# Attention scores of the tail in two parts, other slots for loads and splits, and scores directly behind the transposes in TensorE's order

## The reference

```
attention, batch 4, 8 heads, 576 positions, head width 64:
  cum    = cumsum(max(s, 0))
  scores = q k^T / 8 + min(cum_j - cum_i, 0), masked above the diagonal
  x      = softmax(scores) v                       -> 2304 tokens x 512
first MLP, 512 -> 1024 -> 512:
  h    = x w_in;  solu = h * softmax(h)
  x2   = ((solu - mean) / sqrt(var + 1e-6) * g_ln) w_out
second MLP, 512 -> 2048 -> 512:
  h2   = x2 w2_in;  out = (h2 * clip(h2 + 3, 0, 6) / 6) w2_out
```

## Time and profile before

| | |
|---|---|
| runs | 983.62 and 980.97 us, median 982.3 |
| profiled execution | 981.87 us, its span 980.1 us |
| TensorE busy | 868.6 us (89%), weight loads 772.0 us (79%) |
| VectorE, ScalarE, GpSimd busy | 432.1, 409.5, 309.0 us |
| granted TensorE clock, mean | 0.956 of full speed |
| moved by DMA | 66.60 MB, mean 68 GB/s |

### The profile page before, as it was taken

One profiled execution on the slowest core, in us unless ns is written; L12 is line 12 of the kernel. 1 busy time (PEld: TensorE's weight loads), 2 busy tenths in 40 slices (PEclk: granted clock), 3 DMA queues, 4 the chain that ended last, 5 costly groups with the idle time before them and its releaser, 6 DMA issues.

```text
span 980.1 us, 13896 instructions
## 1 busy us (share of the span) xinstructions
PE 868.6 (89%) x4912; PEld 772.0 (79%) x4912; DVE 432.1 (44%) x1059; ACT 409.5 (42%) x901; POOL 309.0 (32%) x419
## 2 busy tenths in 40 slices
PE   5865778988788998888898899999999999999997
PEld 4654567777777887777887799999999999999996
DVE  3545656656566554666564423223223222222222
ACT  5545655455565454655532324332222222222222
POOL 5884365444563444644426414300000000000000
PEclk9988859999999998999999999999999999999999
DMA  6638223343333333433212204000000000000000
GB/s 186 174 103 220 83 83 93 93 104 99 102 101 92 86 87 105 116 88 97 56 57 74 87 1 129 1 33 1 1 33 1 33 1 1 33 1 1 33 1 32
DMA packets 42724, 66.60 MB, mean 68 GB/s; under 512 B 8032, under 2 KB 20320, under 8 KB 42656
## 3 DMA queue, kind: packets, MB, share of 16 engines
q1 hardware_dynamic: 42656, 65.71, 24.3%
HBM read 60.90 MB, written 4.79 MB: 67 GB/s over the span
## 4 chain that ended last, share of the span: by engine, by line
PE 74%; DVE 8%; issue 6%; ACT 6%; POOL 4%; DMA 1%; SPq 1%; ACTq 0%; DVEq 0%; POOLq 0%
PE psum L737 10%; PE psum L766 7%; PE psum L788 7%; PE psum L786 7%; PE psum L787 7%; PE psum L804 7%; PE psum L805 7%; PE psum L803 7%; PE psum L707 5%; PE psum L682 3%; PE psum L663 3%; PE psum L668 2%; DVE es L944 2%; ACT es L1099 2%; PE psum L750 1%
## 5 line engine op out<-in xcount | busy, mean ns | idle before, releaser
L1011 DVE SCALAR_TENSOR_TENSOR act<-act,psum 128x384 f32<-128x384 f32 x96 | 53.2, 554 | 288.8 <-ACT act L1155 288.8
L1155 ACT ACTIVATE act<-psum,three 128x384 f32<-128x384 f32 x96 | 55.7, 580 | 289.1 <-PE psum L788 289.1
L663 PE MATMUL psum<-qk_hi 128*128 128x128 f32 (+2 forms) x192 | 70.0, 370 | 70.0 <-issue 29.4
L1057 ACT ACTIVATE prob<-prob,nmax 128x128 f32<-128x128 f32 (+4 forms) x144 | 83.6, 581 | 113.1 <-DVE nmax L875 112.9
L786 PE MATMUL psum<-x_hi,w_hi 128*128 128x384 f32 x384 | 130.0, 339 | 0.0
L788 PE MATMUL psum<-x_hi,w_lo 128*128 128x384 f32 x384 | 130.0, 339 | 0.0
L787 PE MATMUL psum<-x_lo,w_hi 128*128 128x384 f32 x384 | 129.5, 337 | 0.0
L805 PE MATMUL psum<-w_hi,g_lo 128*128 128x512 f32 x288 | 113.9, 395 | 0.0
L804 PE MATMUL psum<-w_lo,g_hi 128*128 128x512 f32 x288 | 113.7, 395 | 0.0
L803 PE MATMUL psum<-w_hi,g_hi 128*128 128x512 f32 x288 | 112.0, 389 | 0.0
L547 POOL TENSOR_TENSOR qk_hi<-qk_raw,qk_hi 64x256 fp32r<-64x256 f32 (+1 forms) x64 | 55.9, 873 | 169.2 <-ACT qk_hi L1049 167.7
(11 more groups left out here) (92 smaller groups left out, 1931.4 us busy)
## 6 DMA issues: line engine op xcount, KB each, us to landing
qk_raw<-qk SPq DMA_DIRECT2D x64, 240.0 KB, 4.3
qk_raw<-qk SPq DMA_DIRECT2D x64, 128.0 KB, 2.8
bias<-cum_dram SPq DMA_DIRECT2D x32, 256.0 KB, 3.5
bias_tail<-cum_dram SPq DMA_DIRECT2D x32, 144.0 KB, 4.1
out<-out_sb SPq DMA_DIRECT2D x6, 768.0 KB, 3.5
bias<-cum_dram SPq DMA_DIRECT2D x32, 128.0 KB, 3.2
v_raw<-v_main SPq DMA_DIRECT2D x32, 128.0 KB, 2.2
w_raw<-w_in SPq DMA_DIRECT2D x16, 256.0 KB, 3.2
```

What stands on the lines that cost most here:

```text
L663: pe.matmul(ps, q, qk_hi[p][:, keys], start=(e_ == heads[0]), stop=False)
L1057: sc.activation(p, p, ACT.Exp, scale=-1.0, bias=nmax[:, u % 2, col:col + 1], accum_out=rsum[:, u % 2, col:col + 1]).then_inc(exp_done, 1)
```

## The change

- **Tail in two parts.** `scores` gets a `part`. Part 0 (head 0 of the tail, with the mask, opening the accumulation) is made directly behind the scores of item 2, part 1 (head 1, closing it) in the tail's own place. A new semaphore `tail_half_ready` tells that head 0's tile is free, and its next load waits for that alone.
- **Banks.** Item 2 of a second-kind unit goes to bank 0 in place of 2. Only scores in bank 2 still wait for the last tail's p_lo.
- **Splits.** Head 0 of a unit is split at `BASE - 3`, and at `BASE - 4` for the places 5 to 7; head 1 at `BASE - 2` everywhere (before: `BASE - 1` for the second kind and for place 0).
- **Loads.** Each head's array holds q and k twice in DRAM, so that one DMA fills 128 partitions in place of two of 64; v is padded to 640 rows, so that its second load and VectorE's two memsets go. SyncE issues the loads of q and k ahead of the biases.
- **Orders.** TensorE: transposes, scores, scales, values, then all of the slot's filler in one piece. VectorE: row maximum first, maximum and SOLU of the MLP behind the attention's steps. ScalarE: the MLP's exponential in step 4 and Square in step 5, both ahead of the slot's other work (before: steps 3 and 4, behind it). GpSimd: `widen` a slot later, variance behind the splits of v. The split of x comes up to one slot earlier.

```diff
-S_BANKS = [((2 * (u % PAIRS) + k) % 3,) if FIRST_KIND[u] else ((0,), (1,), (2,), (0,), (1, 2))[k] for u, k in ITEM]
+S_BANKS = [((2 * (u % PAIRS) + k) % 3,) if FIRST_KIND[u] else ((0,), (1,), (0,), (0,), (1, 2))[k] for u, k in ITEM]
...
-    SPLIT_AT.setdefault(BASE[_u] - 3, []).append((_u, 0))
-    SPLIT_AT.setdefault(BASE[_u] - (2 if FIRST_KIND[_u] and _u % (2 * PAIRS) else 1 if _u else 2), []).append((_u, 1))
+    SPLIT_AT.setdefault(BASE[_u] - (3 if _u % (2 * PAIRS) <= PAIRS else 4), []).append((_u, 0))
+    SPLIT_AT.setdefault(BASE[_u] - 2, []).append((_u, 1))
...
-X_AT = {STARTS[t] - 2: t for t in range(NT)}
+X_AT = {max(STARTS[t] - 3, whole_at(t)): t for t in range(NT)}
+SPLIT_X_AT = {n + 1: t for n, t in X_AT.items()}
...
@@ SyncE @@
-                    sp.wait_ge(scores_ready, BASE[u_] + (e_ if FIRST_KIND[u_] else 4) + 1)
+                    if FIRST_KIND[u_] or e_ == 1:
+                        sp.wait_ge(scores_ready, BASE[u_] + (e_ if FIRST_KIND[u_] else 4) + 1)
+                    else:
+                        sp.wait_ge(tail_half_ready, sum(not k for k in FIRST_KIND[:u_ + 1]))
-                for half in (slice(0, DH), slice(DH, P)):
-                    sp.dma_start(qk_raw[p][half, 0:w], src).then_inc(qk_loaded[p], 16)
+                sp.dma_start(qk_raw[p][:, 0:w], (qk1, qk0)[c][head_of(u, e)]).then_inc(qk_loaded[p], 16)
...
@@ TensorE, scores @@
-                if S_BEFORE[n] >= 0:
+                if part != 1 and S_BEFORE[n] >= 0:
                     pe.wait_ge(max_done, TILES_BEFORE[S_BEFORE[n] + 1])
-                    if ITEM[S_BEFORE[n]][1] == 4:
-                        pe.wait_ge(pT_lo_done, LOS_BEFORE[S_BEFORE[n] + 1])
-                    elif 2 in S_BANKS[n] and any(ITEM[m][1] == 4 for m in range(max(0, n - 5), n)):
...
+                if part != 1 and 2 in S_BANKS[n]:
+                    m = max([m for m in range(n) if ITEM[m][1] == 4], default=-1)
+                    wait(pe, pT_lo_done, LOS_BEFORE[m + 1])
...
+                last.then_inc(tail_half_ready if part == 0 else scores_ready, 1)
...
@@ TensorE, the slot @@
             for n in range(-2, END):
+                if 0 <= n < ITEMS:
+                    transpose_probs(n)
+                if 0 <= n + 2 < ITEMS:
+                    k = ITEM[n + 2][1]
+                    if k == 4:
+                        scores(n + 2, 1)
+                    else:
+                        scores(n + 2)
+                    if k == 2:
+                        scores(n + 4, 0)
                 if n in SCALES_AT:
                     scales(SCALES_AT[n])
                 for u, e in SUMS_AT.get(n, ()):
                     weighted_values(u, e)
-                if 0 <= n < ITEMS:
-                    transpose_probs(n)
...
-                if 0 <= n + 2 < ITEMS:
-                    scores(n + 2)
...
```

More of the change, by code:

```diff
@@ L476, in _ @@
             for n in range(-2, BASE[UNITS] + 4):
+                for load in range(3, 2 * UNITS):
+                    u_, e_ = (load - 3) // 2, (load - 3) % 2
+                    if BASE[u_] + (e_ if FIRST_KIND[u_] else 2 * e_ + 2) == n + 2:
+                        load_qk(load // 2, load % 2)
                 for u in range(2, UNITS):
@@ L487, in _ @@
                             load_bias_tail(u)
[L488 to L491, removed]
                 for u in range(2, UNITS):
@@ L620, in _ @@
                     behind = split_v(u, e)
+                if r == 5:
+                    behind = variance(t)
                 for u, e in SPLIT_AT.get(n, ()):
@@ L655, in scores @@
                     diag0 = tile * P
-                    heads = (0, 1) if e is None else (e,)
+                    p = load_of(u, part if e is None else e) % 3
+                    q = qk_hi[p][:, q_at:q_at + P]
                     for lo_, hi_ in [(0, w)] if w <= BANK else [(0, w // 2), (w // 2, w)]:
                         ps = psum[:, at + lo_:at + hi_]
[L659 to L669, removed]
+                        keys = slice(QW[c] + lo_, QW[c] + hi_)
+                        pe.matmul(ps, q, qk_hi[p][:, keys], start=(part != 1), stop=False)
+                        if hi_ > diag0 and part != 1:
+                            mask = mask_tail if e is None else mask_bf
+                            pe.matmul(psum[:, at + diag0:at + hi_], ident_bf[:, :], mask[:, 0:hi_ - diag0],
+                                      start=False, stop=False)
+                        last = pe.matmul(ps, q, qk_lo[p][:, keys], start=False, stop=(part != 0))
+                last.then_inc(tail_half_ready if part == 0 else scores_ready, 1)
             def transpose_probs(n):
@@ L974, in _ @@
                 t, r = STEP_AT.get(n, (None, None))
+                if 0 <= n + 1 < ITEMS:
+                    for tile, e, col in TILES[n + 1]:
+                        row_max(n + 1, tile, e, col)
                 if r == 0 and t >= 3:
                     copy_x2(2 * (t - 3) + 1)
+                if 0 <= n < ITEMS:
+                    split_probs(n)
+                if r == 4 and t >= 2:
+                    copy_x2(2 * (t - 2))
+                if n in SCALES_AT:
+                    scale_pair(SCALES_AT[n])
+                for u, e in SUMS_AT.get(n, ()):
+                    add_parts(u, e)
+                for u in range(UNITS):
+                    if BASE[u + 1] == n:
+                        invert(u)
                 if r == 3:
@@ L1128, in _ @@
                 t, r = STEP_AT.get(n, (None, None))
-                sums = n in SUMS_AT
-                if 0 <= n < ITEMS and not sums:
+                if r == 4:
+                    exp1(t)
+                if r == 5:
+                    square(t)
+                if 0 <= n < ITEMS:
                     copy_probs(n)
```

68 lines of the change are left out of this document (22 added, 46 removed).

## The result

The changed kernel takes 1014.8 us (1014.52 to 1015.12, two runs) against 982.3 us; the ratio is 1.0331, with a 95% interval of 1.027 to 1.0392. The forecast was 944 us with a range of 908 to 984: wrong in sign.

The account below looks back on a forecast made before the run. TensorE's waits, mostly before the scores' first matmuls, were taken to bound the kernel, with GpSimd setting the first 64 us. Terms summed to -38 us, from a median of 982.3 to 944 us; range 908 to 984.

Parts of the forecast that it names:

- G: TensorE's attention slots: scales, values and transposes, behind the scores or waiting for earlier scores' exponentials, wait less: -5 us.
- D: Scores directly behind the transposes lose the cover of other matmuls, so first-kind scores wait for splits: +10 us, bounds 0 and +25.
- E: Items k=2 and k=3 share bank 0, so scores of k=3 wait for k=2's row maximum: +8 us, bounds 0 and +23.
- I: ScalarE's MLP exponential and Square ahead of probabilities' copies, VectorE's maximum and SOLU last, delay attention: +12 us, bounds 0 and +40.
- V: Follow-up theory, not a forecast step: values products behind the scores hold p_hi, making ScalarE's copy and everything behind it late.
- A: Head 0 split one slot earlier for units behind another second-kind unit; most 384-column score waits go: -16.6 us.
- B: Scores no longer wait for the tail's p_lo in bank 1 (512-column form): -10.6 us, bounds -5 and -10.6.
- C: Tail's half 0 in slot k=0 lets head 1 load and split earlier; three waits at batch ends go: -12.2 us.
- F: Projection waits for VectorE's copy shrink: -6 us between 64 and 498 us, -6 us in the stretch without attention.
- H: TensorE's clock between 64 and 498 us: a third of 28 us lost comes back, -10 us, bounds 0 and -22.
- The start: First stretch: two loads less for SyncE and splits a slot earlier, -2 us, bounds 0 and -8.
- the third: Rival, slower: scores' waits for splits or maxima are paid in full, filler queued behind; 1013 us, chance 0.07.

Follow-up runs that it names:

- e14: e9 with ScalarE's copy of the probabilities held, in 15 of the same slots, until TensorE has made the slot's scores: 1004.0 us.
- e9: Changed kernel with only the 16 values products of second-kind units' head 0 moved between transposes and scores: 978.0 us.
- e6: Changed kernel with TensorE's scales and values products moved between transposes and scores, all filler still behind the scores: 946.9 us.
- e13: Changed kernel with item k=2 back in bank 2, the tail's half 0 behind the scores of k=3, and head 1's load a slot later: 997.5 us.
- e8: e2 with item k=2 back in bank 2, the tail's half 0 behind the scores of k=3, and head 1's load a slot later: 925.8 us.
- e2: Changed kernel with TensorE's slot as transposes, scales, values, half the filler, scores, other half of the filler: 927.6 us.
- e10: e2 with the heads' splits in the slots of the kernel before; loads, tail and banks as in e2: 952.6 us.
- e11: e2 with the wait for the tail's p_lo put back before the scores that follow a tail in bank 1: 937.7 us.
- e7: e2 with VectorE's and ScalarE's slots in the order of the kernel before: 955.0 us.
- e5: Changed kernel with TensorE's, VectorE's and ScalarE's orders of the kernel before: 953.8 us (952.9 us with only TensorE's order of before).

## Why the prediction was wrong, step by step

**The step that failed is G.** It counted "scales, values and transposes come behind the scores" as a gain of 5 us. I looked at what TensorE waits for there (the scales' own 4.4 us), and not at what the moved products release: p_hi for ScalarE's copy in the same slot (26 us by e14, with 11 us more in e9), and ScalarE's copy of the products, behind which the conversions of the heads are queued (31 us by e9 against e6 for all remaining products and scales; that this path carries them is read from the trace). The line was in the kernel, `sc.wait_ge(pv_done, 2 * (u - 1) + k // 2 + 1)`, and its wait had cost next to nothing only since the products were the first work of the slot. Moving the products from behind the scores to ahead of them, with nothing else touched, takes 1014.8 to 946.9 us, which is the forecast of 944 within 3 us. That is in part luck: there D costs more than its term, E less, and I is no loss, as below. The shared bank of E takes 17 of these 68 us, but only since the maxima are late (e13 against e8).

**E** had the right place and wait, at 8 us; the scores of k = 3 wait 18.1 us on nmax in the changed kernel, within the bound of 23, and the tail's halves another 5.8, which the step had not foreseen. The size came from V: with the products ahead all nmax waits are 3.2 us (e6), and 0.4 in e2.

**D** was forecast at +10 over the waits of before, for lost cover at the first kind's scores; e6 against e2 measures 19 us for the cover of all scores. By form the first kind waits 31.8 us where the step had 20, again with the late products in it. The first kind's waits in e2 are 6.1 us:

```profile
L668 PE MATMUL psum<-qk_hi 128*128 128x512 f32 x29 | 12.3, 424 | 0.4 <-DVE nmax L884 0.4
...
L668 PE MATMUL psum<-qk_hi 128*128 128x384 f32 x28 | 9.9, 352 | 1.9 <-issue 1.9
...
L668 PE MATMUL psum<-qk_hi 128*128 128x128 f32 x24 | 6.4, 268 | 6.1 <-POOL qk_hi L555 4.5 <-issue 1.6
```

**A, B, C** held, once the products are out of the way. In e2 the 384-column form waits 1.9 us, the 512-column form 0.4, and no wait at a batch's end is over 1.4 us. Steps A and C together (-28.8) measure 25 us (e10), B (-10.6) 10 us (e11); by the ratios, which take out the chip, 28 and 13 us. In the changed kernel the 384-column form is still at 9.4 us; a head's conversion stands behind ScalarE's late copies there, but no run tells this apart.

**F** put 0.65 us on a place: in the changed kernel the wait is 0.61 us at 10 of the 16 places. In the middle stretch the others make it 10.6 us in place of 7 (13.1 before). In the stretch without attention L771's waits fall by 5 us (7.3 to 2.4), but the stretch is only 0.5 us shorter: 2.4 us before L742 for the split of x (0.8 before) and 1.0 us for the norm (L962) stand there now, and TensorE is busy 0.8 us longer. **I** was forecast at +12 and is a gain of 27 us with e2 (e7), and of nothing that can be told with TensorE's order of before (e5). With the changed kernel's own order it was not measured.

**H**, the clock: 0.92 in the middle stretch before and after, 0.95 in e2:

```profile
61.00:448.00 387.00, 346.94 (x2285) 303.80 (x2284) 259.55 (x683) 236.68 (x549) 207.29 (x288) 0.95 0.37 111
```

There TensorE is busy for 346.9 us in place of 359.9 for the same matmuls, so of 47 us gained in this stretch 13 are clock, as far as busy time tells, and 34 are idle time. That is more than the third that I took. The Trainium skill's rule ("TensorE: Matmul & The Clock Gate", HAM oscillation), that waits between groups of matmuls let the clock fall, agrees with this stretch of e2. It doesn't account for the others: in the changed kernel idle time rose by 19 us here without a lower clock, and the first stretch went from 0.92 to 0.88 with 8 us more idle time, but to 0.86 in e2 with 1.8 us more.

**The start** was put at -2; it is +9.5 us. This too hangs on TensorE's order, since e2, which differs from the changed kernel in nothing else, has a start of 61.0 us, 3 us under the kernel before. At 63 us TensorE waits 4.4 us for a head's split, for which GpSimd has pieces of w_in ahead (3.8 us in e2); the products come behind these scores, and ScalarE stands for 9.85 us before its copy at 72.40. How the 9.5 us divide was not tried by itself.

Of the rivals, the third named the right sign and half of the mechanism: waits before the scores with all filler queued behind them (90.5 us in all). It had them as misses of splits and maxima by themselves, where they were made late by the products. Its 1013 us are next to the measured 1014.8, with a sum that fits in part only: its 97 us of idle time in the middle stretch are 93, but of its 14 us for the clock TensorE's busy time shows 5.7, and the 9.5 us of the start were not in it. The signs that were named for a wrong forecast did come: waits before the transposes went from 4.4 to 20.5 us, and idle time behind the start was far over 55 us.

## What to carry to other kernels

When a step moves in one engine's order, list every semaphore that it raises and who waits for it in the same slot, buffers that it frees among them: a wait that costs nothing in the profile of before may do so only because the step came first. Order a slot so that work others wait for comes first (transposes, then what frees their destination), and what waits longest on others, with filler ahead of it. And parts of a change have to be timed in pairs: the orders of VectorE and ScalarE were worth 1 us with one order of TensorE and 27 us with another.

## What the runs showed of the hardware

The largest surprise was the size of one held buffer: 15 copies, started 1.5 us later each (2.9 against 1.4 us behind their transposes, 23 us in sum), cost 26 us of time (e14 against e9). So in this pair of runs about each microsecond of the copies' delay came through at the end. No behaviour of the chip beyond what the prediction used was needed to explain a result.
